# Expert 0's first 128 rows routed by themselves and computed beside the full routing, in a three-layer kernel on one core

## The chip, the cores and the metric

The kernel is one program on one core of a Trainium2 chip. The metric is the device time of that program in microseconds (us). The core has a matrix engine (PE, TensorE), a vector engine (DVE, VectorE), an activation engine (ACT, ScalarE), GpSimd (POOL), and SyncE (SP), which here only issues transfers. Each engine works through its own instructions in order and waits on semaphores for the others.

## The reference

```python
# attention between x (8, 8 heads, 512, 64) and state (8, 8, 32, 64)
xread = softmax(x @ state.T / 8) @ state          # rows of x read the states
sread = softmax(state @ x.T / 8) @ x              # rows of state read x
x = concat([xread, sread], axis=2)                # -> 4608 rows of 512
# experts: each row goes to one of 8, chosen by a cosine
expert_idx = argmax(normalize(x) @ normalize(expert_emb).T / tau, axis=1)
out[mask_e] = gate[mask_e] * (relu(x[mask_e] @ w1[e]) @ w2[e])    # 512 -> 1024 -> 512
# last layer
h = x @ w_in ; g = max(h, 0) + alpha * min(h, 0) ; return g @ w_out    # 512 -> 2048 -> 512
```

## The kernel before, in words

**Attention (0 to 134 us).** Batch by batch (`turn`). Token rows `xrow` leave by SP to the DRAM array `rows_x` (`store_tokens`), four tiles of 128 rows for each of 8 batches, so 32 tiles; the rows read by the states (`copy_srow`, the copy of `ps_sr`) fill the last 2 of the 34 tiles and are also turned and multiplied with the expert embeddings (`turn_tail`, `tail_scores`). The logits of token tiles come along with the reads (`lg0`).

**Routing (134 to 164 us).** For all 34 tiles at once DVE makes the logits `lg`, their maximum, the one-hot choice `onehot`; PE counts (`ps_rank`, `ps_count`); DVE turns counts into a place for every row, and into `place` and `marks`, 0/1 patterns that 34 small products of PE sum up into `ps_idx`: for each slot (128 rows of one expert) which row stands in which lane. From it come `gather_idx` and `scatter_idx`. POOL gathers the rows of a slot from `rows_x` into `xg` by an indirect transfer.

**Experts (164 to 636 us).** A loop over slots (`slot`): PE multiplies the turned rows with w1 (24 products of 512 columns into `ps_h`), DVE copies `ps_h` to `hid`, PE turns it, ACT and DVE split it into a high and a low part (`hT_hi`, and `hidT_lo`, called `rest_hidden` after the change), and PE multiplies with w2 (24 products into `ps_y`). Every product is made of three (`three`: high x high, low x high, high x low), so all operands are split: x by ACT `x_hi` and DVE `x_lo`, weights by `round_chunk` and `rest_chunk`. A weight chunk is 1 MB in `stage`; the semaphore `w_lo_ready` counts split chunks, and expert 0's chunks are numbers 1 to 4. Each slot also turns the next slot's rows (`transpose_x(s + 1)`), gathered by POOL one slot ahead. `scatter` writes results to `rows_y`. The loop bounds come from `table`.

**Last layer (650 us to the end).** `load_y` brings `rows_y` back for a batch, DVE transposes it, the seven products of a fast scheme (`product`) and the down product follow, and `tile` of ACT scales the result by `gate` and SP stores it.

PE runs filler products whose result nobody reads, such as

```python
            pe.wait_ge(w_lo_ready, CH * (E + 1) + 1)
            for _ in range(17):
                pe.matmul(ps_o[0], w_hi[0][:, 0:P], w_hi[0][:, 0:DM], start=True, stop=True)
```

ahead of the last layer. The order on each engine is the order in which the code is written.

## Time and profile before

| | |
|---|---|
| median of 3 runs | 1381.43 us (1380.29 to 1382.03) |
| the profiled execution: its own time | 1380.17 us |
| its span, first to last instruction | 1378.4 us |
| busy share of the span: PE, DVE, ACT, POOL | 97%, 61%, 31%, 12% |
| mean granted clock of TensorE | 0.987 of full speed |

The span is 1.77 us shorter than the time of the same execution. A row of a timeline gives start, duration, engine, line and operation, and in brackets how long the engine sat idle before it and what ended that.

### The profile page before, as it was taken

The page shows a single profiled execution, that of the slowest core. Times are in us where ns is not written, and L with a number is a line of the kernel's source. Part 1 is how long each engine was busy: PE and PEld are TensorE (multiplying, and loading weights), DVE is VectorE, ACT ScalarE, POOL GpSimd, SP SyncE. Part 2 cuts the span into 40 slices and gives each one's busy share as a digit, 9 for nine tenths or more (in the row PEclk, how much of TensorE's full clock was granted, in tenths as well). Part 3 has the DMA queues.
Part 4 walks back from the last instruction along what each step waited for, and adds up shares of the span by engine and source line. Part 5 has one row for each costly group of instructions (what it writes and reads, how often), then busy time and mean ns, then how long its engine had stood idle before and what let it go on. Part 6 is the DMA issues. An engine that isn't in the chain of part 4 may idle for free.

```text
span 1378.4 us, 22418 instructions
## 1 busy us (share of the span) xinstructions
PE 1331.8 (97%) x7774; PEld 1150.0 (83%) x7775; DVE 840.6 (61%) x1085; ACT 424.1 (31%) x610; POOL 165.6 (12%) x228
## 2 busy tenths in 40 slices
PE   8998599999989999997999999999999999999998
PEld 7887488888868888885999999999978888888886
DVE  7897642224464524447677776678965666666552
ACT  6887431113252423235121210122222222222211
POOL 3563021212121122121000000000000000000000
PEclk9999699999999999999999999999999999999999
DMA  7884371113465516244534334443454444444463
GB/s 275 281 283 139 108 252 44 38 46 129 137 243 198 190 46 253 66 140 127 187 131 146 116 118 143 140 137 136 132 139 117 114 114 114 114 114 114 121 117 51
DMA packets 180737, 193.40 MB, mean 140 GB/s; under 512 B 25312, under 2 KB 130784, under 8 KB 180192
## 3 DMA queue, kind: packets, MB, share of 16 engines
q1 hardware_dynamic: 173440, 172.51, 39.8%
q0 software_dynamic: 6112, 19.93, 4.3%
q10 hardware_dynamic: 1152, 0.56, 0.2%
q8 instruction: 16, 0.26, 0.1%
q14 instruction: 17, 0.14, 0.0%
HBM read 125.07 MB, written 67.37 MB: 140 GB/s over the span
## 4 chain that ended last, share of the span: by engine, by line
PE 90%; DVE 6%; issue 1%; ACT 1%; DMA 1%; DVEq 0%; POOL 0%; ACTq 0%; POOLq 0%
PE ps_p L379 13%; PE ps_p L381 13%; PE ps_p L380 13%; PE ps_y L379 5%; PE ps_h L379 5%; PE ps_h L381 5%; PE ps_h L380 5%; PE ps_y L381 5%; PE ps_y L380 5%; PE ps_o L380 5%; PE ps_o L381 5%; PE ps_o L379 5%; PE ps_hT L1567 2%; PE ps_xT L1561 1%; DVE a L1024 1%
## 5 line engine op out<-in xcount | busy, mean ns | idle before, releaser
L379 PE MATMUL ps_p<-b_hi,w_hi 128*128 128x272 f32 x896 | 258.3, 288 | 4.8 <-DVE b_lo L1274 4.8
L381 PE MATMUL ps_p<-b_hi,w_lo 128*128 128x272 f32 x896 | 258.6, 289 | 0.0
L380 PE MATMUL ps_p<-b_lo,w_hi 128*128 128x272 f32 x896 | 258.5, 289 | 0.0
L379 PEld LDWEIGHTS ps_p<-b_hi,w_hi 128*128 128x128 f32 x896 | 168.6, 188 | 5.7 <-DVE b_lo L1274 5.7
L381 PEld LDWEIGHTS ps_p<-b_hi,w_lo 128*128 128x128 f32 x896 | 168.8, 188 | 0.0
L380 PEld LDWEIGHTS ps_p<-b_lo,w_hi 128*128 128x128 f32 x896 | 168.1, 188 | 0.0
L1206 DVE COPY hid<-ps_h 128x512 f32<-128x512 f32 x74 | 51.2, 692 | 176.9 <-PE ps_h L381 171.2
L379 PE MATMUL ps_y<-w_hi,hidT_hi 128*128 128x512 f32 x296 | 123.3, 417 | 0.0
L379 PE MATMUL ps_h<-w_hi,xgT_hi 128*128 128x512 f32 x296 | 121.4, 410 | 1.8 <-DVE xgT_lo L1191 1.8
L1341 DVE SCALAR_TENSOR_TENSOR neg<-gt,alpha 128x2048 f32<-128x2048 f32 x33 | 75.6, 2292 | 71.6 <-DMA gt<-acts 71.6
L1352 DVE TENSOR_TENSOR g_lo<-gt,g_hi 128x2048 fp32r<-128x2048 f32 x34 | 77.9, 2292 | 65.5 <-ACT g_hi L934 65.5
L381 PE MATMUL ps_h<-w_hi,xgT_lo 128*128 128x512 f32 x296 | 117.4, 397 | 0.0
L380 PE MATMUL ps_h<-w_lo,xgT_hi 128*128 128x512 f32 x296 | 117.2, 396 | 0.0
L381 PE MATMUL ps_y<-w_hi,hidT_lo 128*128 128x512 f32 x296 | 116.5, 394 | 0.0
L380 PE MATMUL ps_y<-w_lo,hidT_hi 128*128 128x512 f32 x296 | 116.3, 393 | 0.0
L379 PE MATMUL ps_p<-w_hi,g_hi 128*128 128x512 f32 x272 | 107.5, 395 | 1.3 <-issue 1.3
L381 PE MATMUL ps_o<-w_hi,g_lo 128*128 128x512 f32 x272 | 107.4, 395 | 0.0
L380 PE MATMUL ps_o<-w_lo,g_hi 128*128 128x512 f32 x272 | 107.4, 395 | 0.0
L379 PE MATMUL ps_o<-w_hi,g_hi 128*128 128x512 f32 x272 | 107.4, 395 | 0.0
L380 PE MATMUL ps_p<-w_lo,g_hi 128*128 128x512 f32 x272 | 107.4, 395 | 0.0
L381 PE MATMUL ps_p<-w_hi,g_lo 128*128 128x512 f32 x272 | 107.4, 395 | 0.0
L1210 DVE SCALAR_TENSOR_TENSOR hidT_lo<-ps_hT,hidT_hi 128x512 fp32r<-128x512 f32 x74 | 51.2, 692 | 90.7 <-ACT hidT_hi L846 90.7
(234 smaller groups left out, 2335.4 us busy)
## 6 DMA issues: line engine op xcount, KB each, us to landing
acts<-gb SPq DMA_DIRECT2D x128, 272.0 KB, 2.1
stage<-in_moe_w SPq DMA_DIRECT2D x32, 1024.0 KB, 5.5
gt<-acts SPq DMA_DIRECT2D x32, 1024.0 KB, 6.1
xN_all<-in_xN SPq DMA_DIRECT2D x8, 1024.0 KB, 6.2
rows_x<-xrow SPq DMA_DIRECT2D x32, 256.0 KB, 2.7
out_rows<-orow SPq DMA_DIRECT2D x32, 256.0 KB, 2.0
yz<-rows_y SPq DMA_DIRECT2D x30, 256.0 KB, 3.1
xs_all<-in_xT SPq DMA_DIRECT2D x7, 1024.0 KB, 6.5
```

The source lines that it names most:

```text
L379: pe.matmul(out, s_hi, m_hi, start=start, stop=False)
L380: pe.matmul(out, s_hi, m_lo, start=False, stop=False)
L381: return pe.matmul(out, s_lo, m_hi, start=False, stop=stop)
L1024: dve.tensor_scalar(a2[par][:, g, :], a2[par][:, g, :], cinv[:, g:g + 1], None, ALU.mult)\
L1206: dve.tensor_copy(hid[:, c, :], ps_h[c][:]).then_inc(h_copied, 1)
L1210: dve.scalar_tensor_tensor(out=hidT_lo[:, c, :, :], in0=ps_hT[c][:], scalar=0.0, in1=hidT_hi[:, c, :, :].bitcast(F32), op0=ALU.max, op1=AL ...
L1341: dve.scalar_tensor_tensor(out=neg[:], in0=gt[k % 2][:], scalar=0.0, in1=alpha[:].unsqueeze(2).to_broadcast([P, KFF, P]), op0=ALU.min, op1 ...
L1352: dve.tensor_tensor(g_lo[k % 2][:], gt[k % 2][:], g_hi[k % 2][:].bitcast(F32), ALU.subtract)\
L1561: mm = pe.transpose(ps_xT[:, k, :], xg[:, k * P:(k + 1) * P], ident[:])
L1567: mm = pe.transpose(ps_hT[c][:, k, :], hid[:, c, k * P:(k + 1) * P], ident[:])
```

## The change

It does five things. (1) Expert 0's first 128 rows, looked for among the first 16 tiles (`FT`), get their places from a small routing of their own (`first_hot` to `ps_first`), are gathered at once and taken through both layers as slot 0 outside the loop, between the steps of the full routing; a second gather fetches slot 1. If those tiles held fewer than 128 rows of expert 0, `offset` pushes the later ones to the next slot. (2) Row 0 of `rows_x` is now the row of zeros, and rows start at 1, so that an empty lane's index is 0. (3) The last copy of the state reads (`copy_srow(B)`), the tail's products and two weight splits (`rest_chunk` 2 and 3) change their place. (4) The states of `load_y` come in one transfer instead of four (the other rows still in four), and there are 52 filler products ahead of the last layer with an earlier wait instead of 17. (5) The last four stores go out two by SP and two by ACT instead of four by SP.

```diff
 # SP
-            sp.wait_ge(gathered, 16)
+            sp.wait_ge(gathered, 32)
...
                 for i in quarters:
                     sp.dma_start(yz[i * Q:(i + 1) * Q, 0:S // Q, :], rows[:, :, i * P:(i + 1) * P]).then_inc(y_loaded, 16)
-                    sp.dma_start(yz[i * Q:(i + 1) * Q, S // Q, :], states[:, i * P:(i + 1) * P]).then_inc(y_loaded, 16)
+                if 1 in quarters:
+                    sp.dma_start(yz[:, S // Q, :], states.rearrange("b (i c) -> i b c", i=QB)).then_inc(y_loaded, 16)
...
+            store_tile(XT, 0, [state_row(0, j) for j in range(4)])
+            wait_apart(sp, o_copied, NT + 2)
+            for j in range(2):
+                sp.dma_start(out_v[state_row(1, j):state_row(1, j) + NS, :], orow[j * NS:(j + 1) * NS, 1, :])\
 # POOL
             pool.wait_ge(zero_stored, 16)
-            pool.wait_ge(sr_stored, 16 * B)
             for i in range(SC):
-                pool.wait_ge(x_stored[i], 16 * B)
-            pool.wait_ge(index_ready, 5)
+                pool.wait_ge(x_stored[i], 16 * (FT // SC))
+            pool.wait_ge(gather_ready, 1)
+            pool.indirect_dma_start(xg[:], None, rows_x[:, :],
+                                    bass.IndirectOffsetOnAxis(gather_idx[:, 0:1], 0)).then_inc(gathered, 16)
...
+            pool.wait_ge(xg_read, 1)
+            pool.wait_ge(gather_ready, 2)
             pool.indirect_dma_start(xg[:], None, rows_x[:, :],
-                                    bass.IndirectOffsetOnAxis(gather_idx[:, 0:1], 0)).then_inc(gathered, 16)
+                                    bass.IndirectOffsetOnAxis(gather_idx[:, 1:2], 0)).then_inc(gathered, 16)
 # ACT
+            x_hi(1)
+            act.wait_ge(h_ready, 1)
+            act.activation(hid[:, 0, :], ps_h[0][:], ACT.Copy).then_inc(h_copied, 1)
             act.wait_ge(in_slot_ready, 1)
             act.activation(marks[:, 1, :, :, :], in_slot[:], ACT.Copy, scale=lane[:, 0:1]).then_inc(marks_ready, 1)
+            act.wait_ge(h_ready, 2)
+            act.activation(hid[:, 1, :], ps_h[1][:], ACT.Copy).then_inc(h_copied, 1)
+            for c in range(2):
+                hT_hi(0, c)
             act.wait_ge(norm_clamped, 2)
             act.activation(nrm[:], n2c[:], ACT.Sqrt).then_inc(norm_root, 1)
+            x_hi(2)
...
+            act.wait_ge(o_copied, NT + 2)
+            for j in range(2, 4):
+                r = (QB + j) * TB + S
+                act.dma_start(out_v[r:r + NS, :], orow[j * NS:(j + 1) * NS, 1, :]).then_inc(o_stored[1], 16)
 # DVE
+            rest_chunk(2, 2, 0, 0)
             for k in range(2):
                 dve.wait_ge(tr_copied, 4 * (B - 1) + k + 3)
...
+            copy_srow(B)
             norms(XT, TE, 1)
...
-            rest_chunk(2, 2, 0, 0)
+            logits_x(0, XT - SC)
+            most(0, XT - SC)
+            dve.tensor_tensor(first_hot[:], lg[:, 0:FT, 0], lmax[:, 0:FT], ALU.is_equal).then_inc(first_hot_ready, 1)
             dve.wait_ge(tail_turned, 1)
             dve.tensor_copy(tailT[:, 0, :, :], ps_tailT[:, 0, :, :]).then_inc(tail_copied, 1)
+            dve.wait_ge(first_ranked, 1)
+            step(dve.tensor_tensor_scan(first_incl[:], ps_first_count, zeros[:, 0:FT], 0.0, ALU.add, ALU.add))
+            step(dve.tensor_scalar(first_off[:], first_incl[:, FT - 1:FT], float(P), -1.0, ALU.min, ALU.mult))
+            step(dve.tensor_tensor(first_rank[:], ps_first_rank, first_incl[:], ALU.add))
+            step(dve.tensor_scalar(first_rank[:], first_rank[:], first_off[:, 0:1], None, ALU.add))
+            step(dve.tensor_tensor(first_pos[:], first_rank[:], first_hot[:], ALU.mult))
+            for i in range(2):
+                dve.tensor_tensor(place[:, k, :, :], lanes_below.unsqueeze(1).to_broadcast(half),
+                                  pairs(first_pos[:])[:, k, :].unsqueeze(2).to_broadcast(half), ALU.is_equal)\
+            step(dve.tensor_scalar(offset[:, 0:1], first_off[:], float(P), None, ALU.add))
+            dve.wait_ge(first_summed, 1)
+            step(dve.tensor_scalar(idx_h[:, 0:1], ps_first[:, 0:1], float(P), None, ALU.mult))
+            dve.tensor_tensor(gather_idx[:, 0:1], ps_first[:, 1:2], idx_h[:, 0:1], ALU.add).then_inc(gather_ready, 1)
...
             step(dve.tensor_tensor(excl[:], ps_rank, incl, ALU.add))
+            x_lo(1)
...
+            for c in range(2):
+                rest_hidden(0, c)
             dve.wait_ge(index_summed, 1)
+            step(dve.tensor_scalar(idx_h[:], ps_idx[:, 0, :], float(P), None, ALU.mult))
+            dve.tensor_tensor(gather_idx[:], ps_idx[:, 1, :], idx_h[:], ALU.add).then_inc(gather_ready, 1)
...
+            rest_chunk(3, 3, 1, 0)
...
+            x_lo(2)
...
-            x_lo(1)
-            rest_chunk(3, 3, 1, 0)
 # PE
-                if c == 2:
-                    tail_scores(0)
+            pe.wait_ge(x_copied, SC * (B - 1) + 3)
+            pe.wait_ge(first_hot_ready, 1)
+            pe.matmul(ps_first_rank, lower[:], first_hot[:], start=True, stop=True)
+            pe.matmul(ps_first_count, ones[:], first_hot[:], start=True, stop=True).then_inc(first_ranked, 1)
+            tail_scores(0)
             turn_tail(1)
...
+            for _ in range(8):
+                pe.matmul(ps_h[0][:], w_hi[0][:, 0:P], w_hi[0][:, 0:DM], start=True, stop=True)
...
+            transpose_x(0)
+            pe.wait_ge(w_lo_ready, 2)
+            pe.wait_ge(xT_lo_ready, 1)
+            for c in range(2):
+                hidden(c, range(KD), 0).then_inc(h_ready, 1)
+            for c in range(2):
+                transpose_h(0, c)
             pe.wait_ge(marks_ready, 2)
...
-            for _ in range(14):
-                pe.matmul(ps_h[1][:], w_hi[0][:, 0:P], w_hi[0][:, 0:DM], start=True, stop=True)
+            for c in range(2):
+                pe.wait_ge(hT_lo_ready, c + 1)
+                pe.wait_ge(w_lo_ready, 3 + c)
+                mm = result(c, range(KF // 2), 0)
+            mm.then_inc(y_ready, 2)
+            pe.wait_ge(index_ready, INDEXED)
+            transpose_x(1)
...
-            pe.wait_ge(w_lo_ready, CH * (E + 1) + 1)
-            for _ in range(17):
+            pe.wait_ge(w_lo_ready, CH * E + 1)
+            for _ in range(52):
                 pe.matmul(ps_o[0], w_hi[0][:, 0:P], w_hi[0][:, 0:DM], start=True, stop=True)
```

On PE, from the last token read to the first slot of the loop, the order before (`ps_s` holds counts and tail, `stail` is the tail's rows):

```order
L381 MATMUL ps_x<-stB_hi,a1T_lo 128x264
L1511 MATMUL ps_s<-ident,stail 128x128 x4
L1519 MATMUL ps_s<-embT,a_0 128x8 x4
L1540 MATMUL ps_s<-onehot,lower 128x272
L1541 MATMUL ps_s<-onehot,ones 128x272
L1546 MATMUL ps_x<-marks,place 128x86 x34
L1552 MATMUL ps_h<-w_hi 128x512 x14
L1556 MATMUL ps_y<-w_hi 128x512
L1561 MATMUL ps_xT<-ident,xg 128x128 x4
```

and after:

```order
L395 MATMUL ps_x<-stB_hi,a1T_lo 128x264
L1610 MATMUL ps_turn<-first_hot,lower 128x16
L1611 MATMUL ps_turn<-first_hot,ones 128x16
L1593 MATMUL ps_s<-embT,a_0 128x8 x4
L1585 MATMUL ps_s<-ident,stail 128x128 x4
L1617 MATMUL ps_turn<-first_marks,place 128x2 x16
L1593 MATMUL ps_s<-embT,a_0 128x8 x4
L1648 MATMUL ps_h<-w_hi 128x512 x8
L1652 MATMUL ps_sr<-onehot,lower 128x272
L1653 MATMUL ps_x<-onehot,ones 128x272
L1624 MATMUL ps_xT<-ident,xg 128x128 x4
L393 MATMUL ps_h<-w_hi,xgT_hi 128x512
```

Slot 0's products now stand between the counts and the 34 index products; the two products with `first_hot` and the 16 with `first_marks` are new, and the tail's first product moved behind the last token read.

On DVE, from the end of attention to the first routing step, before:

```order
L1035 TENSOR_TENSOR a_1<-a_1,rinv 128x1024
L1089 TENSOR_SCALAR n2c<-n 128x8
L1092 TENSOR_TENSOR a1T_lo<-ps_turn,a1T_hi 128x512 x2
L1095 RECIPROCAL rtau<-tau 128x1
L1080 RECIPROCAL nrec<-nrm 128x8
L1081 TENSOR_TENSOR nq<-n2c,nrec 128x8
L1082 TENSOR_TENSOR nsum<-nq,nrm 128x8
L1083 TENSOR_SCALAR nden<-nsum 128x8
L1084 RECIPROCAL ninv<-nden 128x8
L1097 TENSOR_SCALAR emb_w<-ninv,rtau 128x8
L970 TENSOR_TENSOR w_lo<-stage,w_hi 128x2048
L1102 COPY srow<-ps_sr 32x512
```

and after:

```order
L1083 TENSOR_TENSOR a_1<-a_1,rinv 128x1024
L1004 TENSOR_TENSOR w_lo<-stage,w_hi 128x2048
L1132 TENSOR_TENSOR a1T_lo<-ps_turn,a1T_hi 128x512 x2
L1135 RECIPROCAL rtau<-tau 128x1
L1019 COPY srow<-ps_sr 32x512
L1122 RECIPROCAL nrec<-nrm 128x8
L1123 TENSOR_TENSOR nq<-n2c,nrec 128x8
L1124 TENSOR_TENSOR nsum<-nq,nrm 128x8
L1125 TENSOR_SCALAR nden<-nsum 128x8
L1126 RECIPROCAL ninv<-nden 128x8
L1138 TENSOR_SCALAR emb_w<-ninv,rtau 128x8
L1143 TENSOR_TENSOR lg<-lg,emb_w 128x224
```

The weight split `w_lo` moved ahead of the last splits of attention, and the copy `srow` ahead of the norms.

DVE after, where the full routing meets slot 0 (`counts` is the running count, `xgT_lo` is `x_lo(1)`):

```order
L1201 SCALAR_TENSOR_TENSOR counts<-ps_x,offset 128x34
L1201 SCALAR_TENSOR_TENSOR counts<-ps_x,zeros 128x34 x7
L1203 TENSOR_TENSOR excl<-ps_sr,counts 128x272
L1159 TENSOR_TENSOR xgT_lo<-ps_xT,xgT_hi 128x512
L1206 TENSOR_SCALAR need_i<-counts 128x8
L1207 TENSOR_SCALAR need_s<-need_i 128x8
L1208 CAST need<-need_s 128x8
```

`xgT_lo`, which stood behind the whole routing, is now in the middle of it, and `need_i` and all places are queued behind it.

## Rows read from the trace of the kernel before

**Rows 1.** The page, busy time, share of the span and instructions of each engine.
```profile
PE 1331.8 (97%) x7774; PEld 1150.0 (83%) x7775; DVE 840.6 (61%) x1085; ACT 424.1 (31%) x610; POOL 165.6 (12%) x228
```
**Rows 2.** Timeline of PE from attention to slot 0.
```profile
129.24 1.97 PE L1440 MATMUL ps_sr<-xN_all,a2T 128*32 128x64 f32 x32
...
136.84 1.06 PE L1519 MATMUL ps_s<-embT,a 128*128 128x8 f32 x8 [2.77 <-DVE a L1105]
...
153.84 2.60 PE L1546 MATMUL ps_x<-marks,place 128*128 128x86 bf16 x34 [7.69 <-DVE place L1151]
...
161.79 0.66 PE L1561 MATMUL ps_xT<-ident,xg 128*128 128x128 f32 x4 [0.89 <-DMA xg<-rows_x,gather_idx]
164.29 0.49 PE L379 MATMUL ps_h<-w_hi,xgT_hi 128*128 128x512 f32 x1 [1.84 <-DVE xgT_lo L1191]
...
165.81 0.63 PE L381 MATMUL ps_h<-w_hi,xgT_lo 128*128 128x512 f32 x1
```
**Rows 3.** Timeline of PE, starts of slot 1 and of the last two slots.
```profile
178.46 0.39 PE L379 MATMUL ps_h<-w_hi,xgT_hi 128*128 128x512 f32 x1
...
610.56 0.40 PE L379 MATMUL ps_h<-w_hi,xgT_hi 128*128 128x512 f32 x1
...
623.10 0.38 PE L1611 MATMUL ps_h<-ident 128*128 128x128 f32 x2
```
**Rows 4.** Timeline of DVE, routing.
```profile
131.62 0.20 DVE L1080 RECIPROCAL nrec<-nrm 128x8 f32<-128x8 f32 x1 [0.72 <-ACT nrm L813]
...
132.71 0.23 DVE L1097 TENSOR_SCALAR emb_w<-ninv,rtau 128x8 f32<-128x8 f32 x1
...
147.28 0.44 DVE L1126 TENSOR_TENSOR excl<-ps_s,counts 128x272 f32<-128x272 f32 x1
...
152.87 2.62 DVE L1151 TENSOR_TENSOR place<-xs_all,lo_b 128x1280 bf16<-128x1280 bf16 x4
...
157.18 0.19 DVE L1167 TENSOR_SCALAR gather_idx<-idx_f 128x43 uint32<-128x43 f32 x1
...
163.30 0.69 DVE L1191 TENSOR_TENSOR xgT_lo<-ps_xT,xgT_hi 128x512 fp32r<-128x512 f32 x1 [1.10 <-ACT xgT_hi L842]
```
**Rows 5.** Timelines and line view, POOL and DVE side by side.
```profile
126.85 1.72 POOL L645 TENSOR_TENSOR stB_lo<-stB,stB_hi 128x528 fp32r<-128x528 f32 x1 [1.30 <-ACT stB_hi L808]
127.33 1.28 DVE L1089 TENSOR_SCALAR n2c<-n 128x8 f32<-128x8 f32 x1
...
98.06 2.99 POOL L645 TENSOR_TENSOR stB_lo<-stB,stB_hi 128x528 fp32r<-128x528 f32 x1 [2.65 <-ACT stB_hi L763]
...
L970 DVE TENSOR_TENSOR w_lo<-stage,w_hi x6: 2281/2284/2292, 67.3 to 188.1; - x4, 128x2048 fp32r<-128x2048 f32 x2
```
**Rows 6.** Timeline of ACT, copy of the last batch's second token tile.
```profile
133.37 0.61 ACT L736 ACTIVATE xrow<-ps_x 128x528 f32<-128x528 f32 x1 [0.57 <-PE ps_x L381]
```
**Rows 7.** The tile xg, transfers of all 39 gathers.
```profile
DMA to landing us min/median/max: 3.3/3.5/6.9
```
**Rows 8.** Windows of 1 us: busy and count of PE, PEld, DVE, ACT, POOL, then PEclk, DMA.
```profile
158.00:159.00 1.00, 1.00 (x5) 0.79 (x4) 0.90 (x4) 1.00 (x1) 0.53 (x1) 0.81 0.00 0
...
168.00:169.00 1.00, 1.00 (x5) 0.83 (x4) 0.08 (x1) 0.10 (x1) 0.00 (x0) 0.69 0.89 352
...
646.00:647.00 1.00, 1.00 (x5) 0.82 (x4) 0.24 (x1) 0.00 (x0) 0.00 (x0) 0.76 0.00 0
```
**Rows 9.** Timelines of PE and DVE between the experts and the last layer.
```profile
641.89 6.29 PE L1648 MATMUL ps_o<-w_hi 128*128 128x512 f32 x17 [5.79 <-DVE w_lo L1248]
650.24 0.40 PE L379 MATMUL ps_p<-b_hi,w_hi 128*128 128x272 f32 x1 [2.05 <-DVE b_lo L1274]
...
647.08 2.50 DVE L1256 STREAM_TRANSPOSE yT<-yz 128x1152 f32<-128x1152 f32 x2 [0.83 <-DMA yz<-rows_y]
```
**Rows 10.** Timeline of SP at the end, and its transfers (KB, us to landing).
```profile
1374.89 1.73 SPq L557 DMA_DIRECT2D out_rows<-orow  x4
...
out_rows<-orow SPq DMA_DIRECT2D x4, 64.0 KB, 1.7
```

More of the change, by code:

```diff
@@ L191, in build @@
         lane = sb("lane", [P, 1], c=ab)
+        first_marks = sb("first_marks", [P, FT, 2], BF16, c=ab)
+        first_hot = sb("first_hot", [P, FT], BF16, c=ab)
+        first_incl = sb("first_incl", [P, FT], c=ab)
+        first_rank = sb("first_rank", [P, FT], c=ab)
+        first_pos = sb("first_pos", [P, FT], BF16, c=ab)
+        first_off = sb("first_off", [P, 1], c=ab)
+        offset = sb("offset", [P, NT], c=ab)
         back_i = sb("back_i", [P, E], I32, c=ab)
@@ L828, in _ @@
             round_chunk(3, 3, 1, 0)
-            act.wait_ge(in_slot_ready, 1)
-            act.activation(marks[:, 1, :, :, :], in_slot[:], ACT.Copy, scale=lane[:, 0:1]).then_inc(marks_ready, 1)
-            act.wait_ge(norm_clamped, 2)
-            act.activation(nrm[:], n2c[:], ACT.Sqrt).then_inc(norm_root, 1)
-            act.wait_ge(gate_diff, 1)
-            act.activation(ld[:], ld[:], ACT.Exp).then_inc(gate_exp, 1)
-            act.wait_ge(index_ready, 5)
-            for i in range(SC):
-                act.wait_ge(x_stored[i], 16 * B)
-            act.wait_ge(sr_stored, 16 * B)
             def x_hi(n):
@@ L854, in _ @@
             x_hi(1)
+            act.wait_ge(h_ready, 1)
+            act.activation(hid[:, 0, :], ps_h[0][:], ACT.Copy).then_inc(h_copied, 1)
+            act.wait_ge(in_slot_ready, 1)
+            act.activation(marks[:, 1, :, :, :], in_slot[:], ACT.Copy, scale=lane[:, 0:1]).then_inc(marks_ready, 1)
+            act.wait_ge(h_ready, 2)
+            act.activation(hid[:, 1, :], ps_h[1][:], ACT.Copy).then_inc(h_copied, 1)
+            for c in range(2):
+                hT_hi(0, c)
+            act.wait_ge(norm_clamped, 2)
+            act.activation(nrm[:], n2c[:], ACT.Sqrt).then_inc(norm_root, 1)
+            x_hi(2)
+            act.wait_ge(gate_diff, 1)
+            act.activation(ld[:], ld[:], ACT.Exp).then_inc(gate_exp, 1)
+            act.wait_ge(index_ready, INDEXED)
+            for i in range(SC):
+                act.wait_ge(x_stored[i], 16 * B)
+            act.wait_ge(sr_stored, 16 * B)
+            act.sem_inc(yrow_ready, 1)
             with act.Fori(0, E // 2) as pair:
@@ new lines, in x_lo, with rest_hidden @@
+            def x_lo(n):
+                dve.wait_ge(xT_hi_ready, n)
+                dve.tensor_tensor(xgT_lo[:], ps_xT[:], xgT_hi[:].bitcast(F32), ALU.subtract).then_inc(xT_lo_ready, 1)
+            def rest_hidden(s, c):
+                dve.wait_ge(hT_hi_ready, 2 * s + c + 1)
+                dve.scalar_tensor_tensor(out=hidT_lo[:, c, :, :], in0=ps_hT[c][:], scalar=0.0,
+                                         in1=hidT_hi[:, c, :, :].bitcast(F32), op0=ALU.max,
+                                         op1=ALU.subtract).then_inc(hT_lo_ready, 1)
```

178 lines of the change are left out of this document (98 added, 80 removed).

## Prediction

> **What bounds the kernel now.** I read the page first: PE is busy 97% of the span [rows 1], so time can only come from the few places where PE waits or does work nobody reads. PE's timeline shows one large such place, from the end of attention to slot 0 [rows 2]. PE last works densely at 134 us, waits 2.77 us, then 7.69 us, runs 34 small index products, fills with products nobody reads, waits for the gather, and begins slot 0 at 164.29. The waits name DVE: its routing steps follow one another from the logits to the places (end of `place` 152.87 + 2.62 = 155.49) and `gather_idx` (157.18 + 0.19 = 157.37) [rows 4]. Then the gather lands at 161.79 [rows 2]. Behind that come turn and split, and slot 1 begins at 178.46 [rows 3]; a slot with nothing in its way takes 623.10 - 610.56 = 12.54 us [rows 3]. Two smaller places are the way from the last slot to the last layer and the last stores; I come to them below.
>
> What the change must do is plain then: let PE have slot 0 behind it while DVE still routes. The figure to compare is the start of slot 1, 178.46 before.
>
> **When the first rows arrive.** All times are on the scale of the trace of before. PE's last read of the states ends at 129.24 + 1.97 = 131.21 [rows 2]; the copy `srow` now runs next on DVE, to 131.95 (0.67 us). The norms and `emb_w` took 131.62 to 132.94 [rows 4], 1.32 us, so they end at 133.3. Logits and maximum of 28 tiles are two operations of 224 elements, nearer to the 0.44 us of 272 [rows 4] than to the 0.2 of a small one: 0.8 us, then `first_hot` 0.2: 134.3. PE's last token read stood behind a tail product that waited for DVE until 136.84; now it needs only ACT's copy that ends at 133.37 + 0.61 = 133.98 [rows 6], and with 1.1 us for its six products ends at 135.1; the two count products take 0.3. DVE then has five steps at 0.22 (1.32 us for six of them in rows 4) = 1.1, to 136.5; two patterns of 1,024 elements, where 4,352 took 2.62 [rows 4], 0.62 each, to 137.7; `offset` 0.2 and the tail copy 0.7, to 138.6, under which PE's 16 sums of two columns lie; two steps: `gather_ready` at 139.1. Before, from the end of `gather_idx` (157.37) to the landing (161.79) it was 4.4 us [rows 2, 4]: 143.5. SP issues its last row stores and expert 1's first chunk about 4 us sooner than before, so this gather meets a chunk in flight, where before it had the queues to itself. Gathers took 3.3 at least and 6.9 at most [rows 7], so contention costs 0 to 3.6 us; I take 0.5, near the low end, since the median is 3.5. The gather lands at 144.0.
>
> One move speaks against this sum. `rest_chunk(2)` now starts at 127.33 on DVE, beside POOL's `stB_lo`. The rows show two things [rows 5]: an 8-element operation of DVE took 1.28 us there and ended when POOL did, and POOL's `stB_lo` took 2.99 us beside another `rest_chunk`, while none of six `rest_chunk` was longer than 2.292. So I let POOL pay: `stB_lo` ends near 129.8 and PE needs it at 131.2, at no cost. The other bound is that DVE waits for POOL's 1.2 us, PE's reads start 1.0 late, and slot 1 is up to 1.0 later. The Trainium skill, GPSIMD Engine Reference, Specifications, says that GpSimd shares its SBUF interfaces with VectorE, with contention for DVE instructions with two SBUF inputs as well; it does not say who waits. By the side that hurts, the sum below would be 1.0 smaller.
>
> **What waits for it.** Call the landing G = 144.0. The new wait is DVE's `x_lo(1)`, and `need_i`, all places and thus the second gather are queued behind it. Before it DVE is done early: four choices of 28 tiles (1.7), the last tiles (1.4), counts and `excl` (2.3 with PE's part) lead from 139.1 to 144.5, and in before `excl` ended at 147.72 [rows 4]. `x_lo` ended 163.99 - 161.79 = 2.2 after the landing, so G + 2.2 = 146.2: DVE waits 1.0 us and gives 0.7. Its places then take 155.49 - 147.72 = 7.8: done at 154.0, 1.5 sooner than before.
>
> PE begins slot 0's products at G + 2.5 (164.29 - 161.79 [rows 2]) = 146.5. Then 24 products. At the full clock one takes 0.233 (12.54 us of a slot hold 48 of them and 12 turns), at half 0.427 (512 columns at 1.2 GHz; the product at 165.81 lasts 0.63 [rows 2] where that at 178.46 lasts 0.39 [rows 3]): 5.6 or 10.2 us. PE has done little since 139, and in before the granted clock was at half each time that PE had idled, and returned in the windows at 158, 168 and 646 us [rows 8], which is 4.3 to 4.6 us after PE began dense work at 153.84, 164.29 and 641.89 [rows 2, 9] (in slot 0 it first fell on the way; the long product of 165.81 is that). So I charge 4.5 x 0.45 = 2.0: the products end at 154.1. The Trainium skill, TensorE: Matmul & The Clock Gate, Part 1, says that the throttled state is the default and that activity releases it; the trace agrees, and by it the eight fillers ahead are too few to hold the clock over the wait that follows.
>
> Then ACT's copy (0.75 with its hand-over) and the turns (0.6): 155.4. The 34 index products took 2.60 [rows 2]; now all places are ready: 157.8. DVE: two steps to `gather_idx`, 158.2; three more and `rest_chunk(3)`, 0.65 + 2.28 [rows 5], 161.1. PE: the first half of layer 2 under that, the second half waits for this split (`w_lo_ready` 4) and takes 12 x 0.233 = 2.8: 164.0. The second gather (158.2 + 4.4 = 162.6) has landed; turns 0.66, then x's split, 1.84 idle [rows 2] as before slot 0: slot 1 at 166.5. That is **12.0 us** sooner than 178.46. DVE's gate work (4 us) now lies beside PE's layer 2, and its end must come before slot 1's first copy, 2.8 us after the start; there is room. SP holds expert 1's chunks 2 and 3 until the second gather is in (162.6, before 161.79), which 12 more slots of expert 0 hide. Without that cover (an expert 0 of two slots) it would cost several us.
>
> **No extra slot.** The reference's inputs (seed 0) send 1,536 of the first 2,048 rows to expert 0, so `offset` is 0 and the number of slots stays 37.
>
> **To the last layer.** DVE's transpose waited 0.83 us for the rows [rows 9] and was otherwise free at 646.25. With one states transfer in place of four, SP issues three and ACT two instead of four each; the last was issued at 641.57. Up to 0.83 can go, DVE being next; I take **0.8** (bounds 0 and 0.83). Of the fillers, 52 x 0.233 = 12.1 us from 635.9 end at 648.0, where the 17 ended before (641.89 + 6.29), since these run at once at the full clock. PE then still waits for `b_lo` (650.24 less 0.8) [rows 9]: cost 0.
>
> **The end.** Four stores were issued in 1.73 us and the last landed 1.7 later [rows 10]. Two and two save two issues: **0.8** (bounds 0.4, if ACT's issues are slower, and 0.9). New constants at the start lie under the first loads.
>
> Sum: 12.0 + 0.8 + 0.8 = 13.6 off the execution's own 1380.17: 1366.6. The median lies 1.26 above that execution, so **1367.8 us**.
>
> **Rivals.**
> *The clock stays full* through attention's end and the fillers: 2.0 more, 1365.8. For it speaks that PE's 2.77 us wait is gone; against, some 5 us with little work before 146.5. Chance 0.13.
> *The first gather is late*, up to the 6.9 of rows 7: 3.1 more than I took, and DVE's and PE's chains both shift by it: up to 1370.9. Chance of more than 1 us: 0.12.
> *Half clock through all of slot 0*, because the small waits inside it keep it down: 24 x 0.194 = 4.7 in place of 2.0, and 4.7 in layer 2, 7.4 together: 1375.2. Against it: 4.5 us of dense work sufficed three times. Chance 0.08.
> *Nothing gained*: fewer than 128 rows of expert 0 in 16 tiles, a 38th slot of 12.5 us: 1380.3. Chance 0.02.
> *Slower*: the same wait at `x_lo(1)`, with the gather held behind all that SP has queued. Each us late is a us of the kernel; from 13.6 us it decides the sign. A landing 18 us late (162) gives 1385.8. Against it: none of 39 gathers took over 6.9. Chance 0.03.
> My forecast has the rest, 0.62, with its own range 1365.5 to 1370.
>
> **The numbers.** The range 1364.5 to 1373 takes in the forecast, the full clock and the late gather, 0.87, and leaves out the other three. A measurement of this kernel can tell about 0.2% (2.8 us) from no change. Faster by more: 0.62 + 0.13 + 0.12 + 0.08 = 0.95, less 0.01 for a sum of small misses: 0.94. Within: 0.03. Slower: 0.03.
>
> **What the profile would show.** The first xg transfer lands near 144 and DVE waits about 1 us at `xgT_lo`; PE starts slot 0 near 146.5 with granted clock at half for some 4 us; `w_lo` ends near 161 with PE waiting for it; slot 1 starts near 166.5; DVE's wait before `yT` is about 0; four stores issue in 0.9 us. I would be wrong if the landing were after 147, if the clock stayed down past 152, or if PE's wait in the loop grew.

## The result and the profile after

After the change the kernel takes 1374.25 us, median of 5 runs (1372.04 to 1374.68); before, on the same chip, 1382.03 (1380.29 to 1382.52). The ratio is 0.9943, 95% interval 0.9933 to 0.9954: faster, by 7.8 us. I had forecast 1367.8 with a range up to 1373.0; the sign was right, and of 13.6 us some 5.8 did not come. In the profiled executions, which the lines below show, it is 5.3.

The page after, busy time by engine: TensorE has barely more work than in [rows 1].
```profile
PE 1337.0 (98%) x7820; PEld 1152.7 (84%) x7821; DVE 842.8 (62%) x1106; ACT 424.6 (31%) x611; POOL 166.6 (12%) x228
```
The timeline of PE after, from attention to slot 3 (start, length, and in brackets the idle time ahead and what ended it):
```profile
131.94 0.36 PE L393 MATMUL ps_turn<-stB_hi,a1T_hi 128*128 128x264 f32 x1 [0.94 <-DVE a1T_lo L1132]
...
140.02 3.15 PE L1648 MATMUL ps_h<-w_hi 128*128 128x512 f32 x8
...
144.11 0.66 PE L1624 MATMUL ps_xT<-ident,xg 128*128 128x128 f32 x4 [0.46 <-DMA xg<-rows_x,gather_idx]
146.34 0.48 PE L393 MATMUL ps_h<-w_hi,xgT_hi 128*128 128x512 f32 x1 [1.57 <-DVE xgT_lo L1159]
...
153.37 1.54 PE L1666 MATMUL ps_x<-marks,place 128*128 128x88 bf16 x34
...
159.21 0.47 PE L393 MATMUL ps_y<-w_hi,hidT_hi 128*128 128x512 f32 x1 [0.83 <-DVE w_lo L1004]
...
164.81 1.09 PE L1624 MATMUL ps_xT<-ident,xg 128*128 128x128 f32 x4 [2.57 <-DMA xg<-rows_x,gather_idx]
167.38 0.80 PE L393 MATMUL ps_h<-w_hi,xgT_hi 128*128 128x512 f32 x1 [1.48 <-DVE xgT_lo L1159]
...
182.06 0.40 PE L393 MATMUL ps_h<-w_hi,xgT_hi 128*128 128x512 f32 x1
...
189.28 0.66 PE L1624 MATMUL ps_xT<-ident,xg 128*128 128x128 f32 x4 [1.03 <-DMA xg<-rows_x,gather_now]
```
Read it against [rows 2, 3]. Slot 0 now stands where the routing was, and its first product comes at 146.34 instead of 164.29. Slot 1 starts at 167.38 instead of 178.46, 11.1 us sooner. But two waits carry the name of a gather: 2.57 us ahead of slot 1 and 1.03 ahead of slot 3's turn. Slot 1 lasts 182.06 - 167.38 = 14.68 us, where a free slot takes 12.5.

The timelines of DVE and POOL, the same stretch, and PE's turn of the hidden rows at the end:
```profile
126.63 1.71 POOL L665 TENSOR_TENSOR stB_lo<-stB,stB_hi 128x528 fp32r<-128x528 f32 x1 [1.31 <-ACT stB_hi L833]
127.08 3.40 DVE L1004 TENSOR_TENSOR w_lo<-stage,w_hi 128x2048 fp32r<-128x2048 f32 x1
...
145.50 0.69 DVE L1159 TENSOR_TENSOR xgT_lo<-ps_xT,xgT_hi 128x512 fp32r<-128x512 f32 x1 [0.27 <-ACT xgT_hi L856]
...
156.00 0.20 DVE L1246 TENSOR_TENSOR gather_idx<-ps_x,idx_h 128x44 uint32<-128x44 f32 x1
156.77 2.29 DVE L1004 TENSOR_TENSOR w_lo<-stage,w_hi 128x2048 fp32r<-128x2048 f32 x1
156.98 2.91 POOL L715 DMA_INDIRECT xg<-rows_x,gather_idx  x1 [15.72 <-DVE gather_idx L1246]
...
169.05 0.37 DVE L1268 RECIPROCAL gate<-gsume 128x34 f32<-128x34 f32 x1
172.88 0.69 DVE L1287 COPY hid<-ps_h 128x512 f32<-128x512 f32 x1 [3.47 <-PE ps_h L395]
...
173.63 0.66 PE L1630 MATMUL ps_hT<-ident,hid 128*128 128x128 f32 x4
```
The chain of waits, the second gather from its instruction to its landing, and under it the tile xg, all 39 gathers:
```profile
156.98 7.69 DMA xg<-rows_x,gather_idx
```
```profile
DMA to landing us min/median/max: 3.3/3.6/7.7
```
This gather took 7.69 us to land, 3.28 before; it is the slowest of all, where the slowest had been 6.9 [rows 7]. PE's own windows of 1 and 2 us say what moved meanwhile (length, PE busy and count, granted clock, DMA share, GB/s):
```profile
162.00:163.00 1.00, 0.24 (x2) 1.00 1.03 422
163.00:164.00 1.00, 0.00 (x0) 1.00 0.99 401
165.00:167.00 2.00, 0.90 (x4) 0.50 0.28 105
169.00:171.00 2.00, 2.00 (x7) 0.50 0.45 158
```
The DMA engines are full with SP's next weight chunk (SP issued it at 159.15, as soon as the split of expert 0's last chunk had ended at 159.06), PE is idle, and when x arrives the granted clock is at half: it is there from 164.6 to 171.5.

The stretch from experts to last layer, and the end, after:
```profile
627.99 12.06 PE L1738 MATMUL ps_o<-w_hi 128*128 128x512 f32 x52
642.71 0.59 PE L393 MATMUL ps_p<-b_hi,w_hi 128*128 128x272 f32 x1 [2.65 <-DVE b_lo L1348]
...
639.54 2.50 DVE L1330 STREAM_TRANSPOSE yT<-yz 128x1152 f32<-128x1152 f32 x2 [1.16 <-DMA yz<-rows_y]
...
1366.59 0.69 ACT L981 ACTIVATE orow<-ps_p,gate 128x512 f32<-128x512 f32 x1 [10.51 <-PE ps_p L395]
1367.30 0.88 ACTq L996 DMA_DIRECT2D out_rows<-orow  x2
1367.34 0.78 SPq L616 DMA_DIRECT2D out_rows<-orow  x2
```
DVE still waits for the rows, 1.16 us where it was 0.83 [rows 9]. The end, from the start of the last `orow` to the end of the span (1370.1), takes 3.51 us; before 4.27.

A ledger of both profiled executions: how much sooner each milestone comes than before. The last product of the experts is the last `ps_y` of layer 2. Group 0 is the first batch of the last layer; its first product waits for `b_lo`, which DVE makes from the transposed rows `yT`.

| milestone | before | after | sooner |
|---|---|---|---|
| slot 1, first product | 178.46 | 167.38 | 11.08 |
| slot 2, first product | 190.98 | 182.06 | 8.92 |
| last product of the experts | 635.48 | 627.62 | 7.86 |
| group 0, first product | 650.24 | 642.71 | 7.53 |
| last `orow` starts | 1374.13 | 1366.59 | 7.54 |
| end of span | 1378.4 | 1370.1 | 8.3 |

So the loss has places: 0.9 at slot 1's start, 2.2 in slot 1, 1.1 until the experts end, 0.3 at the rows for the last layer where 0.8 was to be gained.

### The profile page after: what moved, and what is told of

Read it like the earlier page. It is cut to its first block, busy times and chain, and to the rows that moved or that the text cites. A ratio compares the mean times of both kernels' runs of the same rounds, so it can differ in the third digit from the quotient of the medians.

```text
span 1370.1 us, 22457 instructions
## 1 busy us (share of the span) xinstructions
PE 1337.0 (98%) x7820; PEld 1152.7 (84%) x7821; DVE 842.8 (62%) x1106; ACT 424.6 (31%) x611; POOL 166.6 (12%) x228
## 4 chain that ended last, share of the span: by engine, by line
PE 90%; DVE 6%; DMA 2%; issue 1%; ACT 1%; DVEq 0%; POOL 0%; SPq 0%; ACTq 0%; POOLq 0%
PE ps_p L393 13%; PE ps_p L395 13%; PE ps_p L394 13%; PE ps_y L393 5%; PE ps_y L395 5%; PE ps_y L394 5%; PE ps_h L393 5%; PE ps_h L395 5%; PE ps_h L394 5%; PE ps_o L394 5%; PE ps_o L393 5%; PE ps_o L395 5%; PE ps_hT L1630 2%; PE ps_xT L1624 1%; DVE a L1066 1%; PE ps_sr L1514 1%
## 5 line engine op out<-in xcount | busy, mean ns | idle before, releaser
L1287 DVE COPY hid<-ps_h 128x512 f32<-128x512 f32 x72 | 49.8, 691 | 171.5 <-PE ps_h L395 166.3
```

What stands on the lines that cost most here:

```text
L1287: dve.tensor_copy(hid[:, c, :], ps_h[c][:]).then_inc(h_copied, 1)
```

## The experiments

Each is an edit on the kernel after; 7 and 8 stand on top of edit 3. Ratios are to the kernel before as measured beside each, with the 95% interval, which is 1.5 to 2 us to either side: smaller differences are read from the timelines alone. The interval of the kernel after, 0.9933 to 0.9954, overlaps with those of edits 1 and 3, and lies clear of those of 7 and 8.

### 1. The weight chunk held back (e1_chunk_held)
```diff
-            for i in range(2):
-                load_weights(CH + i, i, expert_chunk(1, i), 3 + i)
+            load_weights(CH, 0, expert_chunk(1, 0), 3)
             sp.wait_ge(gathered, 32)
+            load_weights(CH + 1, 1, expert_chunk(1, 1), 4)
```


> Changed kernel with one edit: SP loads expert 1's second weight chunk only when the second gather has landed. In the changed kernel that gather's instruction on POOL takes 2.91 us and the rows land 4.9 us behind its end. Theory A (the gather is late for two reasons, the chunk of 1 MB that SP starts at 159.1 and DVE's weight split beside POOL): the landing follows the end of POOL's instruction by 2.2 us again, the instruction itself stays at 2.9; the gather lands near 162.2, just as PE ends slot 0's products (162.2), PE's wait of 2.57 us goes, the clock stays full in slot 1, the kernel is 3.5 to 4.5 us faster than the changed one. Rival B (the gather is slow of itself, its rows being spread over the array, and the chunk does nothing to it): landing still 4.9 us behind, time within 1 us of the changed kernel or slower.

1372.02 us, ratio 0.9924 (0.9910 to 0.9938). Timeline, e1:
```profile
159.56 2.90 POOL L715 DMA_INDIRECT xg<-rows_x,gather_idx  x1 [17.61 <-DVE gather_idx L1246]
164.98 0.63 PE L1624 MATMUL ps_xT<-ident,xg 128*128 128x128 f32 x4 [0.17 <-DMA xg<-rows_x,gather_idx]
...
173.36 0.66 PE L1630 MATMUL ps_hT<-ident,hid 128*128 128x128 f32 x4 [1.35 <-DVE hid L1287]
```
With the queues to itself the gather lands 2.4 us after the end of its instruction, 4.8 in the kernel after (164.67 - 159.89); PE's wait for it falls from 2.57 to 0.17 and slot 1 runs at full clock. The instruction itself still takes 2.90. And slot 1 still lasts 14.21 us: a wait for DVE's `hid`, 1.35, has come up. The time is 2.2 us less than the 1374.25 of the kernel after, and not 3.5 to 4.5: that wait is one part of what is missing, and slot 0's first layer at half clock for 3.4 us (149.0 to 152.4) another.

### 2. The split held behind the gather by a semaphore (e2_dve_held)
```diff
                                     bass.IndirectOffsetOnAxis(gather_idx[:, 1:2], 0)).then_inc(gathered, 16)
+            pool.sem_inc(gather_issued, 1)
...
+            dve.wait_ge(gather_issued, 1)
             rest_chunk(3, 3, 1, 0)
```


> Changed kernel with one edit: DVE starts the split of expert 0's last weight chunk only after POOL has passed the instruction of the second gather. Theory A: POOL's instruction takes 1.06 us again instead of 2.91, ends near 158.0, the split runs 158.1 to 160.4, SP's chunk starts behind it at 160.4 and hardly meets the gather, which lands near 161; PE's second half of layer 2 ends near 163.3, 1 us later than now, and slot 1 starts near 165.7 with the clock full: 3 to 4 us faster than the changed kernel. Rival C (the length of POOL's instruction has nothing to do with DVE): it still takes 2.9 and slot 1 starts no sooner than in the changed kernel (167.4), the time is the same or 1 us slower.

1375.53 us, 0.9954 (0.9940 to 0.9968): no gain. Timelines, e2:
```profile
158.59 2.29 DVE L1006 TENSOR_TENSOR w_lo<-stage,w_hi 128x2048 fp32r<-128x2048 f32 x1
158.76 2.95 POOL L716 DMA_INDIRECT xg<-rows_x,gather_idx  x1 [17.51 <-DVE gather_idx L1248]
```
The run did not test what it was for. The semaphore behind the DMA instruction passed before the instruction had begun its work, so the split still lay beside it, and POOL still took 2.95. Slot 0 ran at half clock here until 151.1, which the kernel after did not in its profiled execution.

### 3. The split moved ahead (e4_split_early)
```diff
             choice(XT - SC, NT)
+            rest_chunk(3, 3, 1, 0)
             dve.wait_ge(ranks_ready, 1)
...
             dve.tensor_tensor(scatter_idx[:], idx_f[:], empty[:], ALU.add).then_inc(index_ready, 2)
-            rest_chunk(3, 3, 1, 0)
```


> Changed kernel with one edit: the split of expert 0's last weight chunk stands on DVE ahead of the wait for the counts, where DVE idles 1.3 us, and so ends near 145. Theory A: all of DVE's chain is 1.1 us later from there, the second gather's instruction starts near 158.1 with DVE doing only small work (1.1 us), SP's chunk is long in (146 to 152), the gather lands near 162.5; PE no longer waits for the split and ends layer 2 near 161.5; slot 1 starts near 165, clock full: 3.5 to 4.5 us faster than the changed kernel, and this would be the version to keep. Rival B or C: landing stays near 166, the time is the same or slower.

1371.46 us, 0.9927 (0.9914 to 0.9941). Timelines of POOL, PE and DVE, e4:
```profile
160.01 0.95 POOL L715 DMA_INDIRECT xg<-rows_x,gather_idx  x1 [18.66 <-DVE gather_idx L1247]
164.26 0.60 PE L1624 MATMUL ps_xT<-ident,xg 128*128 128x128 f32 x4
166.35 0.49 PE L393 MATMUL ps_h<-w_hi,xgT_hi 128*128 128x512 f32 x1 [1.48 <-DVE xgT_lo L1159]
...
172.61 0.66 PE L1630 MATMUL ps_hT<-ident,hid 128*128 128x128 f32 x4 [1.81 <-DVE hid L1287]
...
168.02 0.37 DVE L1268 RECIPROCAL gate<-gsume 128x34 f32<-128x34 f32 x1
171.87 0.69 DVE L1287 COPY hid<-ps_h 128x512 f32<-128x512 f32 x1 [3.48 <-issue]
```
The instruction takes 0.95 us instead of 2.91, the chunk has moved before the gather, x waits for PE, not PE for x. From `gather_idx` to slot 1 it is 7.1 us, where the kernel after needs 11.2 (156.20 to 167.38). But slot 1 lasts 14.66, as long as in the kernel after although its clock is full: DVE ends the gates at 168.39, and its first instruction inside its loop comes 3.48 us later, with nothing that the profile names between. PE waits 1.81 us for it. The time is 2.8 us less than that of the kernel after, where 3.5 to 4.5 was expected.

### 4. The states in four transfers, as before (e5_states_four)
```diff
-                if 1 in quarters:
-                    sp.dma_start(yz[:, S // Q, :], states.rearrange("b (i c) -> i b c", i=QB)).then_inc(y_loaded, 16)
+                    sp.dma_start(yz[i * Q:(i + 1) * Q, S // Q, :], states[:, i * P:(i + 1) * P]).then_inc(y_loaded, 16)
```
(and two of the four by ACT, for group 0, as before, with the waits to match.)

> Changed kernel with one edit: the states of each batch come back in four small transfers as before, not one. I had counted the one transfer as 0.8 us gained; in the changed kernel DVE waited 1.16 us for the rows where it had waited 0.83 before. Theory D (the single transfer, whose descriptors SP writes in 0.74 us behind the two others, lands last): four transfers give the same time or up to 0.4 us less. Rival E (it did help, and the rest is the scatter or noise): this is 0.5 to 0.8 us slower than the changed kernel.

1374.28 us, 0.9948 (0.9934 to 0.9961), beside 0.9943: no difference that the time could tell. DVE's wait ahead of `yT` is 1.10, where the twelve profiled executions with one transfer show 1.16 (the kernel after) to 1.79. From the last product of the experts to group 0 it is 15.02 us here, 15.09 to 15.73 in those twelve, and 14.76 before. So one transfer instead of four shows no gain; whether it costs up to 0.7 us, one execution with four cannot show.

### 5. The last stores by one queue, as before (e6_stores_sp)
```diff
-            for j in range(2):
+            for j in range(4):
...
-            act.wait_ge(o_copied, NT + 2)
-            for j in range(2, 4):
-                r = (QB + j) * TB + S
-                act.dma_start(out_v[r:r + NS, :], orow[j * NS:(j + 1) * NS, 1, :]).then_inc(o_stored[1], 16)
```


> The kernel after, with the last four stores all issued by SyncE as before the change (four in a row) instead of two by each of two queues. Theory H (the two stores in a row cost 0.76 us, as the ends of the two traces show: 4.27 us from the last copy to the end before, 3.51 after): from the last copy to the end 4.2 to 4.3 us, and the time 1375.0 (1374.25 + 0.76). Rival (the landing, not the issue, sets the end): 3.5 to 3.7 us and 1374.2.

1376.51 us, 0.9962 (0.9948 to 0.9975). Queue of SP at the end, e6:
```profile
1369.27 1.72 SPq L616 DMA_DIRECT2D out_rows<-orow  x4
```
Four issues again take 1.72 us, and from `orow` (1368.51) to the end (1372.7) it is 4.19 us instead of 3.51: 0.68 us for the two queues. The median is 2.3 above that of the kernel after, more than its end explains; the milestones up to the experts' end are the same to 0.1 us (slot 1 at 167.33, last product 627.53). Of the 2.5 us between the two profiled executions, 1.5 lie behind the start of group 0 (see 9).

### 6. The split of chunk 2 put back (e9_chunk2_back)
```diff
-            rest_chunk(2, 2, 0, 0)
             for k in range(2):
                 dve.wait_ge(tr_copied, 4 * (B - 1) + k + 3)
...
             step(dve.tensor_scalar(emb_w[:], ninv[:, XT:TE], rtau[:, 0:1], None, ALU.mult))
+            rest_chunk(2, 2, 0, 0)
```


> The kernel after, with the rest of chunk 2 put back behind the scale emb_w, where it stood before the change. What the change's move of it was worth: the reads of the last pass no longer wait for VectorE's 3.40 us at GpSimd's port (0.94 us at 131.94, so they start at about 131.0), but the split (2.3 us) now stands in the chain of the routing and its first gather comes 1.3 to 1.6 us later, since xrow must be copied and stored too. Theory G (the routing's chain sets slot 0, as forecast): slot 1 starts 1 to 1.6 us later than after's, 1375.3 to 1376. Rival (the wait of 0.94 is what the reads and with them the end of all stores cost, and the routing has slack): 1373.2 to 1374.

1375.18 us, 0.9951 (0.9938 to 0.9965). No idle time stands ahead of the reads now: their first product is at 130.66. But slot 0 begins 18.1 us behind it (148.73), where in the kernel after it is 14.4 (131.94 to 146.34), and slot 1 starts at 170.39. So the move ahead costs the reads 0.9 and spares the routing more. In the time the difference (0.9951 beside 0.9943 and 0.9948 for the kernel after) is too small to be told.

### 7. Products between the turns and the hidden layer of slot 0 (e7_fill_slot0)
```diff
             transpose_x(0)
+            for _ in range(6):
+                pe.matmul(ps_h[0][:], w_hi[0][:, 0:P], w_hi[0][:, 0:DM], start=True, stop=True)
```
On top of the split moved ahead.

> The kernel after, with the rest of chunk 3 split ahead of the wait for the ranks (as in the split-early experiment, 1371.46 us), and six more 512-column products into ps_h[0] between the transposes of slot 0 and its hidden layer. Theory E (the clock of slot 0 is worth some 2 us, and it falls because TensorE stands idle for 2.3 us between the transposes and the first product of the hidden layer): the six products fill that gap, the hidden layer runs at full clock, 140 to 160 reads about 0.9 instead of 0.75, the index products stand 1.5 to 2 us sooner, slot 1 starts near 164.5, and the time is 1369.5 to 1370.0. Rival (slot 0 is not what sets slot 1: the places on VectorE are, or VectorE in slot 1 takes the gain as a longer wait for hid): the clock is full and the time stays within 0.7 us of 1371.5. Rival 2 (the clock fell earlier, in 138 to 140, and stays down whatever stands in the later gap): the products run at half clock, end after xgT_lo is ready, and the time is 0.5 to 1 us more than 1371.5.

1370.31 us, 0.9910 (0.9896 to 0.9924), beside 0.9927. Layer 1 of slot 0 takes 5.7 us (147.26 to 152.92) where it took 8.5 in e4 (147.39 to 155.86), and slot 1 starts at 164.01. In slot 1 PE waits for `hid` 1.80 us, as in e4. The intervals of e4 and e7 overlap, so the gain itself is read from the timeline.

### 8. The gates ahead of x (e8_gate_early)
```diff
             norms(0, NT + E, 2)
-            x_lo(2)
             step(dve.tensor_tensor(ld[:, 0:XT, :], ld[:, 0:XT, :], ninv[:, 0:XT].unsqueeze(2).to_broadcast(to_x),
...
             dve.reciprocal(gate[:], gsume[:]).then_inc(gate_ready, 1)
+            x_lo(2)
```
(the same on ACT: the exponential ahead of `x_hi(2)`), on top of the split moved ahead.

> The kernel after, with the rest of chunk 3 split ahead of the wait for the ranks (1371.46 us), and the gates computed before x_lo(2) on VectorE and x_hi(2) on ScalarE, where both stood idle for 3.4 and 4.6 us. Theory F (in slot 1 TensorE waited 1.81 us at 172.61 for hid because VectorE entered its loop only after the gates: it was 3.48 us at nothing that the profile names between the last gate instruction at 168.4 and hid at 171.87): with the gates done by 165.7 the entry into the loop starts at about 166.3 instead of 168.4, the wait for hid falls to about 0, and the time is 1369.6 to 1370.2. Rival (the entry waits for something else, such as ScalarE's or the queue's side of the loop): the wait stays, 1371 to 1372.

1367.78 us, 0.9898 (0.9884 to 0.9911). Timelines of DVE and PE, e8:
```profile
162.56 0.37 DVE L1267 RECIPROCAL gate<-gsume 128x34 f32<-128x34 f32 x1
164.06 0.69 DVE L1159 TENSOR_TENSOR xgT_lo<-ps_xT,xgT_hi 128x512 fp32r<-128x512 f32 x1 [1.14 <-ACT xgT_hi L856]
167.91 0.69 DVE L1287 COPY hid<-ps_h 128x512 f32<-128x512 f32 x1 [3.16 <-PE ps_h L395]
...
169.11 0.60 PE L1630 MATMUL ps_hT<-ident,hid 128*128 128x128 f32 x4
```
Now DVE waits for PE's product (3.16) and not PE for DVE; slot 1 lasts 12.78 us, slot 2 12.54. That is 1.88 us less for slot 1 than in e4, and the edit's own work. Slot 1 also starts 1.54 sooner than in e4 (164.81), which is mostly the clock: slot 0's first layer took 7.22 us, in e4 8.47. So a part of the step from e4 to e8 is luck with the clock.

### 9. All three, and the clock ahead of group 0 (e10_all, e11_all_fill62, e12_fill17, e13_after_again)
e10 is 7 and 8 together. e11 adds one line to it, e12 puts 17 into the same line on the kernel after, e13 is the kernel after once more.
```diff
-            for _ in range(52):
+            for _ in range(62):
                 pe.matmul(ps_o[0], w_hi[0][:, 0:P], w_hi[0][:, 0:DM], start=True, stop=True)
```


> The three edits together, on the kernel after: the rest of chunk 3 split ahead of the wait for the ranks, six more products between the transposes and the hidden layer of slot 0, and the gates computed before x_lo(2) and x_hi(2). The gates alone brought the early split from 0.9927 to 0.9898 of before, the six products alone to 0.9910. Theory (the two are different pieces: the clock in slot 0, and the entry of VectorE into its loop in slot 1): slot 1 starts at about 164.0 at full clock, no wait for hid in it, and the time is 1366.0 to 1367.0, or 0.988 to 0.989 of before. Rival (VectorE's entry into the loop then ends later than the first hidden half of an earlier slot 1, so the six products buy nothing): within 0.5 us of 1367.8.

> The same three edits, and 62 instead of 52 idle products ahead of group 0 of the second layer pair. In the kernel after TensorE stands idle for 2.65 us behind the 52 products and group 0 begins at full clock, falls to half at about 642.8 and comes back at 645.9; in the kernel before, with 17 products run late, group 0 is at full clock. Theory I (that half-clock stretch costs 1 to 2 us of the second pair's start): the idle gap falls to 0.5 us, no half clock in group 0, and the time is 1 to 1.5 us below the run with 52. Rival (group 0's first products wait for VectorE and ScalarE in any case): within 0.4 us of the run with 52.

> The kernel after with 17 idle products ahead of group 0 instead of 52, that is this part of the change undone. The forecast costed it at nothing. Theory I (clock in group 0): with 17 products TensorE is idle for some 10.7 us ahead of group 0 (632.0 to 642.7), group 0 starts at half clock and stays there for longer than in the kernel after (3.1 us there): 1 to 2 us slower than the kernel after of the same call. Rival (nothing, as forecast): within 0.5 us.

> The kernel after, unchanged, on the chip of this call, so that the three others have it beside them: 0.9943 of before as on record (1374 to 1375 us), with slot 0 at full clock in the profiled run in one of two cases, 1372 us, and at half clock in the other, 1374 to 1374.7.

| kernel | us | ratio (95%) | slot 1 | last product of experts | group 0 | group 0 to the last `orow` |
|---|---|---|---|---|---|---|
| e13, after | 1373.85 | 0.9948 (0.9934 to 0.9962) | 167.33 | 627.82 | 643.44 | 725.42 |
| e12, 17 products | 1374.63 | 0.9956 (0.9943 to 0.9970) | 169.97 | 629.38 | 645.08 | 725.47 |
| e10, all | 1367.05 | 0.9897 (0.9882 to 0.9912) | 164.32 | 621.20 | 636.80 | 725.64 |
| e11, all, 62 | 1367.44 | 0.9901 (0.9886 to 0.9916) | 164.61 | 621.59 | 637.32 | 725.38 |

e10 is not measurably faster than e8 (0.9898), although its experts end 1.6 us sooner (622.81 in e8): 0.95 of that is lost again behind the start of group 0, where e8 takes 724.69 us and e10 725.64. Windows of 1 us, e13 (length, PE busy and count, granted clock, DMA share, GB/s):
```profile
645.00:646.00 1.00, 1.00 (x6) 0.50 1.04 399
647.00:648.00 1.00, 0.94 (x6) 1.00 1.04 371
650.00:651.00 1.00, 1.00 (x6) 0.50 1.09 414
652.00:653.00 1.00, 1.00 (x7) 0.50 1.03 372
```
The clock falls twice: it is at half from 642.9 to 646.3, as group 0 begins, and again from 649.7 to 653.1. The profiled execution of the kernel after has only the first fall (642.5 to 645.9). From group 0 to the last `orow` that execution takes 723.88 us, before, at full clock, 723.89, e2 723.87 and e9 723.90, both with one fall like it. e4 and e8, at half clock until 7 us into group 0, take 724.58 and 724.69; e1, e5, e6, e7, e10, e11, e12 and e13, with half clock until 9 to 10 us into it, take 725.38 to 725.69. So half clock in the first 3.5 us of group 0, where PE waits for `b_lo` anyway, costs nothing, and half clock after it up to 1.8. It also shows how the 1372.04 of the profiled execution stands to the median of 1374.25: e13's, 1374.31, has the same slot 1 to 0.05 us, group 0 0.73 later and 1.54 more behind it. And it is why e11 gains nothing: with its 62 products the clock stays full until 643.5, and it falls then, until 646.9. With 17, PE is idle for 11.21 us and the clock is at half from 637.1 to 654.2; that costs the same 1.5 behind group 0's start as in e13, and not more. Why the second fall comes in one execution and not in another, no run shows.

## Why the prediction was right or wrong

**When the first rows arrive**: right. The gather landed at 144.1 (said 144.0), and the new wait at `x_lo(1)` is 0.27 us (said 1.0), so the rival on the slower side had nothing behind it. The side step was wrong: I let POOL pay for `rest_chunk(2)` beside `stB_lo`. POOL took its 1.71 us, DVE's split 3.40 for 2.28, and PE waited 0.94 at 131.94. The two rows of [rows 5] show the rule that I did not draw from them: whoever starts first keeps its time, and the other one is lengthened and ends behind it. Before the change, DVE had begun first at 97.59 (POOL's operation of 98.06 ended 1.18 us behind it, less than the 1.72 that it takes alone), and POOL at 126.85 (`n2c` ended with it). The Trainium skill, SBUF — State Buffer, SBUF: two separate sides, says just this: an exclusive lock for the whole instruction, by who starts first. By that rule DVE pays, and the trace agrees: 128.34 (end of `stB_lo`) + 2.14 = 130.48 (end of the split). The forecast had named this bound, and 1.0 was its price.

**Slot 0**: the sum had 2.0 for half clock, and the sentence behind it held the eight fillers for too few. In the profiled execution of after, and in e6 and e13, the clock was back at 144.2 to 144.5, before slot 0, and its layer 1 ran in 5.7 us at full clock. In e1, e2, e4, e5, e8, e9 and e12 it took 7.2 to 8.5. Both ways happen. The rival of a full clock would have ended at 1365.8, and did not, for the next reason. In the profiled execution this was luck that hid part of the miss: at full clock the sum would have put slot 1 14.0 us sooner, and it came 11.1 sooner. So 2.9 us were lost there, of which the ledger shows 0.92. Where slot 0 ran at half clock and nothing else was mended (e2, e5, e12), slot 1 starts at 169.2 to 170.0. (The sum also has a slip of 0.2: 155.4 + 2.60 is 158.0.)

**What failed: "the second gather (158.2 + 4.4 = 162.6) has landed".** It was the step that carried the largest error. `gather_idx` ended at 156.20, earlier than said, and the gather landed 8.5 us later, not 4.4. Two things were added, each shown by an experiment:
- DVE's `rest_chunk(3)` starts 0.2 us ahead of POOL's DMA instruction, which then takes 2.90 to 2.95 us in all eight kernels that have the two side by side, and 0.95 or 0.96 in all five (e4, e7, e8, e10, e11) that have the split ahead. In the kernel before, the split lay 5 us behind it, and it took 1.06. The split ends at 159.06 and the instruction 0.83 later, as if it had waited for the split and then done its own work. e1 keeps the split beside it and takes only the chunk away, and the instruction still takes 2.90: it is the split. The Trainium skill, SBUF — State Buffer, Who interferes with whom, says that a `tensor_tensor` did not stall descriptor writing where that was measured; here, beside an indirect DMA, it does, and the measurement decides. That the reading of the indices is what waits would fit the page's rule on reads; no run here separates it.
- SP's 1 MB chunk fills the DMA engines from 161 to 164; without it the landing takes 2.4 instead of 4.8 us behind the instruction (e1).

The trace of before had shown both. Its slowest gather, the 6.9 us of [rows 7] that I read as contention of transfers, is the one below; it began beside a split, and the DMA engines were full behind it (share 0.98 and 1.03 from 192 to 194). Timelines of DVE and POOL, before:
```profile
188.12 2.28 DVE L970 TENSOR_TENSOR w_lo<-stage,w_hi  x1
188.19 3.09 POOL L681 DMA_INDIRECT xg<-rows_x,gather_now  x1 [0.79 <-POOL gather_now L679]
```

I had seen contention for the first gather and priced it, and gave the second one its old 4.4, though the change moved a split and a chunk onto it. PE was idle for 2.57 us, and slot 1 ran at half clock until 171.5; in e1, with a wait of 0.17, it ran at full clock.

**What also failed: "its end must come before slot 1's first copy, 2.8 us after the start; there is room".** The gates ended 2.0 us after slot 1's start, but DVE's first instruction in its loop comes another 3.5 us later, which I did not count: `hid` comes 5.5 us after the start, where in a free slot it comes 3.0 us after it. This loss was hidden under the first. At half clock PE reaches that point just then, so that the profile of after shows no wait there; when e1 and e4 gave the clock back, the wait came up, 1.35 and 1.81 us, and slot 1 stayed at 14.2 to 14.7 us. With the split and the gates moved both (e8) it is 12.78; the gates alone were not tried. Before, the gates were done at 162.2, ahead of all slots.

**Until the experts end**: 1.1 us, nearly all of it the wait of 1.03 at 189.28 for slot 3's rows. It is gone in e1, e4, e5, e8, e10 and e11, and there in e2, e6, e7, e9, e12 and e13. Where it is there, that gather took 6.1 to 6.3 us to land; where it is gone 3.3 to 4.5, or 5.7 in e1, where it began 4 us sooner. In the kernel after it began at 183.00 and the DMA engines were full from 186 to 189 (share 0.99 to 1.05) with a weight chunk. That fits a gather beside a chunk once more, but no run isolates it, so the cause stays open.

**To the last layer**: the term of 0.8 was wrong. DVE's wait grew to 1.16, and e5 with four transfers has the same time. I had taken the number of issues for what sets the landing. In the chain of waits, after:
```profile
633.17 6.34 DMA yz<-rows_y
```
The transfer issued at 633.17 is the single one of the states; it lands last, at 639.51, 7.3 us after the first issue (632.25). Before, the last of four, issued at 641.57, landed 7.0 us after the first (640.11), and in e5 it is 7.2. So fewer issues did not bring the last landing forward. The fillers at nothing: 0.8 us in e12, within what can be told, and in part slot 0's clock.

**The end**: forecast 0.8, in the profile 0.76, and 0.68 by e6.

With the sizes from the ledger (the first of them net of the 2.0 that the clock gave back): 13.6 - 0.92 (slot 1's start) - 2.16 (slot 1) - 1.06 (up to the experts' end) - 1.13 (0.8 forecast and 0.33 lost at the rows) = 8.33, against 8.3 measured in the span.

A version that beats both kernels is e8 at 1367.78 (0.9898), or e10 at 1367.05, beside the 1373.85 of the kernel after that was measured with e10 (ratio of the two 0.995).
